# A seven-product MLP: the first batch's tokens one step earlier, and another order of the products in a unit

## The reference

```python
# attention, 8 heads of 64: local window |i-j| < 16, plus 24 block summaries (max of k, mean of v)
a = softmax([mask(q k^T / 8), q k_sum^T / 8 + log 32]);  x = a @ [v, v_sum]
# gated convolution ("MoE" in the names): w_in 512 x 1024, 3 taps, w_out 1024 x 512
h = relu(x @ w_in);  c = conv3(h, conv_w) over tokens;  x = (h * sigmoid(c)) @ w_out
# layer norm and MLP: w_ch1 512 x 2048, w_ch2 2048 x 512
xn = (x - mean) / sqrt(var + 1e-6) * g_ln;  out = x + relu(xn @ w_ch1) @ w_ch2
```

## Time and profile before

| | |
|---|---|
| median of three runs | 494.68 us |
| profiled execution | 494.09 us |
| its span, first to last instruction | 492.4 us |
| TensorE busy | 472.2 us (96%), 2807 matmuls |
| VectorE busy | 288.1 us (59%) |
| ScalarE busy | 213.8 us (43%) |
| GpSimd busy | 275.3 us (56%) |
| chain that ended last | TensorE 80%, VectorE 10% |

### The profile page before, as it was taken

How to read it: one execution, slowest core, us unless ns; L and a number is a source line. 1 busy time by engine, 2 the same in 40 slices (tenths; PEclk the granted TensorE clock), 3 DMA queues, 4 the chain that set the end, 5 groups by cost and what they waited for, 6 DMA issues and landing times.

```text
span 492.4 us, 7970 instructions
## 1 busy us (share of the span) xinstructions
PE 472.2 (96%) x2807; PEld 416.4 (85%) x2807; DVE 288.1 (59%) x616; ACT 213.8 (43%) x516; POOL 275.3 (56%) x413
## 2 busy tenths in 40 slices
PE   7978899999999999997999999999999999999996
PEld 7866777898989898876889898888998988888985
DVE  6498987488756785898655334165573334243324
ACT  3878988834334545634434234333410313231310
POOL 3447788999801300577786787784005187787300
PEclk9999999999999999999999999999999999999999
DMA  9999981121100200000120222022020022102003
GB/s 221 222 236 209 225 204 57 47 85 47 40 0 1 86 1 0 1 0 28 60 87 4 82 86 86 2 86 85 2 107 23 0 87 85 62 25 88 0 1 128
DMA packets 62115, 35.63 MB, mean 72 GB/s; under 512 B 48064, under 2 KB 55004, under 8 KB 61788
## 3 DMA queue, kind: packets, MB, share of 16 engines
q1 hardware_dynamic: 60508, 34.72, 25.6%
q10 hardware_dynamic: 1568, 0.39, 0.4%
HBM read 31.08 MB, written 3.15 MB: 70 GB/s over the span
## 4 chain that ended last, share of the span: by engine, by line
PE 80%; DVE 10%; SPq 3%; issue 2%; POOL 2%; DMA 1%; ACT 1%; DVEq 0%; POOLq 0%
PE two L1375 10%; PE two L1377 9%; PE two L1376 9%; PE two L1352 7%; PE two L1355 7%; PE two L1354 7%; PE two L1215 4%; PE two L1217 4%; PE two L1216 4%; PE two L1281 4%; PE two L1282 4%; PE two L1283 4%; PE two L1167 2%; PE two L1156 2%; DVE h L778 2%
## 5 line engine op out<-in xcount | busy, mean ns | idle before, releaser
L1375 PE MATMUL two<-wv,h 128*128 128x512 f32 x192 | 77.0, 401 | 2.9 <-DVE h L778 2.7
L1355 PE MATMUL two<-combo,wa 128*128 128x384 f32 x224 | 75.6, 337 | 0.0
L1352 PE MATMUL two<-combo,wa 128*128 128x384 f32 x224 | 75.5, 337 | 0.0
L1354 PE MATMUL two<-combo,wa 128*128 128x384 f32 x224 | 75.3, 336 | 0.0
L1377 PE MATMUL two<-wv,h 128*128 128x512 f32 x192 | 75.2, 392 | 0.0
L1376 PE MATMUL two<-wv,h 128*128 128x512 f32 x192 | 75.2, 392 | 0.0
L582 POOL TENSOR_TENSOR wa<-wst,wa 128x256 fp32r<-128x256 f32 x39 | 31.4, 835 | 54.4 <-ACT wa L1006 54.4
L540 POOL TENSOR_TENSOR wa<-asum,wa 128x256 fp32r<-128x256 f32 x52 | 44.6, 859 | 4.3
L1375 PEld LDWEIGHTS two<-wv,h 128*128 128x128 f32 x192 | 36.0, 188 | 13.0 <-DVE h L778 6.6
L546 POOL TENSOR_TENSOR asum<-wst 128x256 f32<-128x256 f32 x26 | 22.9, 881 | 43.0 <-PE two L1355 32.0
L851 DVE TENSOR_TENSOR u<-two,u 128x384 f32<-128x384 f32 x16 | 8.9, 558 | 64.9 <-PE two L1355 64.9
(11 more groups left out here) (120 smaller groups left out, 1041.8 us busy)
## 6 DMA issues: line engine op xcount, KB each, us to landing
wst<-in_moe_w_ch SPq DMA_DIRECT2D x26, 512.0 KB, 3.4
vW<-in_v SPq DMA_DIRECT2D x16, 240.0 KB
kn<-in_k SPq DMA_DIRECT2D x15, 192.0 KB, 4.0
qn<-in_q SPq DMA_DIRECT2D x15, 192.0 KB, 3.7
out<-y SPq DMA_DIRECT2D x11, 256.0 KB, 2.0
vblk<-in_v SPq DMA_DIRECT2D x3, 768.0 KB, 6.4
wst<-in_moe_w_in SPq DMA_DIRECT2D x8, 256.0 KB, 3.5
wst<-in_moe_w_out SPq DMA_DIRECT2D x8, 256.0 KB, 2.9
```

Source lines behind the costliest of these rows:

```text
L1352: nc.tensor.matmul(o, wk[:, 0, kk], ck[:, 0, kk], start=(first and kk == 0), stop=False, skip_group_check=True)
L1354: nc.tensor.matmul(o, wk[:, 0, kk], ck[:, 1, kk], start=False, stop=False, skip_group_check=True)
L1355: ins = nc.tensor.matmul(o, wk[:, 1, kk], ck[:, 0, kk], start=False, stop=(kk == 1), skip_group_check=True)
L1375: nc.tensor.matmul(o, hi, vh, start=(f == 0 and c == 0), stop=False, skip_group_check=True)
```

## The change

The first batch's tokens are transposed in steps 11 and 12, not 12 and 13; centring stands in front of gate(10). The first batch's token sums are VectorE's, in step 12, and its `combo` tiles are spread over steps 12 to 14, with a wait of its own for `combo3`. In a unit TensorE's order becomes products 0 to 2, tiles 0 to 2, products 3 and 4, tiles 3 to 5, products 5 and 6; in the last unit tiles 3 to 5 stand behind product 6. `h2_low(g, 1)` stands in front of the sum of `p1`; tokens of the second batch are behind tiles 1 and 2; `stats`, `copy_y`, the second batch's `combo` tiles and `add_out` move to fit.

```diff
--- before.py
+++ after.py
@@ -65,12 +65,12 @@
         COLS_STEP = GPP * (NPAIR - 2)
 
 
-        TOK_TILE = {12: {0: 0, 1: 1, 3: 2, 4: 3}, 13: {0: 4, 1: 5, 3: 6, 4: 7}}
-        TOK_UNIT = {2: {3: 0, 4: 1}, 3: {3: 2, 4: 3}, 4: {3: 4, 4: 5}, 5: {3: 6, 4: 7}}
+        TOK_TILE = {11: {0: 0, 1: 1, 3: 2, 4: 3}, 12: {0: 4, 1: 5, 3: 6, 4: 7}}
+        TOK_UNIT = {2: {1: 0, 2: 1}, 3: {1: 2, 2: 3}, 4: {1: 4, 2: 5}, 5: {1: 6, 2: 7}}
         NSLOT = 2 * KD
 
 
-        COMBO_ORDER = [(0, 2, 6, 3, 1, 4, 5), (0, 1, 2, 3, 4, 5, 6)]
+        COMBO_ORDER = [(0, 2, 6, 1, 3, 4, 5), (0, 1, 2, 3, 4, 5, 6)]
         SUMS = {3: ((1, 0),), 4: ((1, 1),), 6: ((2, 0),), 9: ((2, 1),), 12: ((3, 0),), 15: ((3, 1),)}
         place = [0]
 
@@ -551,13 +551,6 @@
 
                     pool.wait_ge(x_done, NG)
                 elif l == 1:
-                    for i in range(4):
-                        out, in0, in1, op = token_sum(i)
-                        if i == 0:
-                            pool.wait_ge(xr_done, NSLOT)
-                        else:
-                            pool.wait_ge(tsum_done, i)
-                        nc.gpsimd.tensor_tensor(out, in0, in1, op).then_inc(tsum_done, 1)
 
                     pool.wait_ge(h_ready, 4 * KF)
                 elif l == 2:
@@ -787,23 +780,24 @@
             for s in range(2 * KF):
                 if s >= 1:
                     taps(s)
+                    if s == KF + 2:
+                        inverse_std(0)
+                        dve.wait_ge(rstd_done, 1)
+                        for i in range(T):
+                            centre(0, i)
                     gate(s)
                 if s == KF + 1:
                     for i in range(T):
                         stats(i)
-                if s == KF + 2:
-                    inverse_std(0)
-                    dve.wait_ge(rstd_done, 1)
-                    for i in range(T):
-                        centre(0, i)
-                if s == 2 * KF - 3:
+                elif s == KF + 4:
+                    token_sums(0, range(4))
+                elif s == KF + 5:
                     for k in COMBO_ORDER[0][0:3]:
                         combo_low(0, k)
-                if s == 2 * KF - 2:
-                    for k in COMBO_ORDER[0][3:5]:
+                elif s == KF + 6:
+                    for k in COMBO_ORDER[0][3:6]:
                         combo_low(0, k)
-            for k in COMBO_ORDER[0][5:7]:
-                combo_low(0, k)
+            combo_low(0, COMBO_ORDER[0][6])
 
             dve.wait_ge(hg_done, 2 * KF)
             for g in range(NU):
@@ -811,27 +805,33 @@
                 dve.wait_ge(p1_done, g + 1)
                 dve.wait_ge(prod_done, NPROD * g + 2)
                 nc.vector.tensor_tensor(u2[:], b, p1[:], ALU.add).then_inc(u2_done, 1)
-                if g == 1:
-                    for i in range(4):
-                        stats(T + i)
-                elif g == 2:
+                if g == 2:
                     inverse_std(1)
                     dve.wait_ge(rstd_done, 2)
                     for i in range(3):
                         centre(1, i)
+                elif g == NFP + 1:
+                    add_out(5)
+                h2_low(g, 0)
+                if g == 1:
+                    for i in range(4):
+                        stats(T + i)
                 elif g == 6:
                     token_sums(1, (0, 1))
                 elif g == NFP - 1:
-                    combo_low(1, 0)
-                    combo_low(1, 1)
+                    for k in range(3):
+                        combo_low(1, k)
                 elif g == NFP:
-                    for k in (4, 5, 6):
-                        combo_low(1, k)
-                elif g == NFP + 1:
-                    add_out(5)
-                h2_low(g, 0)
+                    combo_low(1, 5)
+                    combo_low(1, 6)
+                    add_out(0)
+                    add_out(1)
                 dve.wait_ge(prod_done, NPROD * g + 4)
                 nc.vector.tensor_tensor(u3[:], b, p1[:], ALU.add).then_inc(u3_done, 1)
+                dve.wait_ge(prod_done, NPROD * g + 5)
+                dve.wait_ge(u3_done, g + 1)
+                nc.vector.tensor_tensor(u3[:], a, u3[:], ALU.add).then_inc(c22_done, 1)
+                h2_low(g, 1)
                 if g == 1:
                     for i in range(4, T):
                         stats(T + i)
@@ -841,21 +841,18 @@
                 elif g == 6:
                     token_sums(1, (2, 3))
                 elif g == NFP - 1:
-                    combo_low(1, 2)
                     combo_low(1, 3)
+                    combo_low(1, 4)
                 elif g == NFP:
-                    for n in range(5):
+                    for n in range(2, 5):
                         add_out(n)
-                dve.wait_ge(prod_done, NPROD * g + 5)
-                dve.wait_ge(u3_done, g + 1)
-                nc.vector.tensor_tensor(u3[:], a, u3[:], ALU.add).then_inc(c22_done, 1)
                 dve.wait_ge(prod_done, NPROD * g + 6)
                 nc.vector.tensor_tensor(p1[:], b, p1[:], ALU.add).then_inc(c21_done, 1)
                 dve.wait_ge(prod_done, NPROD * g + 7)
                 dve.wait_ge(u2_done, g + 1)
                 nc.vector.tensor_tensor(u2[:], a, u2[:], ALU.add).then_inc(c12_done, 1)
-                for k in (1, 2, 3):
-                    h2_low(g, k)
+                h2_low(g, 2)
+                h2_low(g, 3)
             for n in range(T, NTT):
                 add_out(n)
 
@@ -986,6 +983,8 @@
                     act.wait_ge(prod_done, NPROD * (NFP * b - 1) + k + 1)
                 elif k == 5:
                     act.wait_ge(h_ready, 4 * KF)
+                elif k == 3:
+                    act.wait_ge(h_ready, 2 * (KF + 6))
                 else:
                     act.wait_ge(tile_proj, T * (KF + 3))
                 nc.scalar.copy(combo[k][:, 0], combo_src(k)).then_inc(ch_done, 1)
@@ -1040,6 +1039,8 @@
                 at_tile = TOK_TILE.get(s, {})
                 if s >= 1:
                     tap0(s)
+                    if s == KF + 2:
+                        root(0)
                     for i in (0, 1, 3):
                         if i in at_tile:
                             tokens(0, at_tile[i], ps_h[at_tile[i] % 2])
@@ -1052,16 +1053,13 @@
                 if s == KF + 1:
                     for n in range(T):
                         copy_y(n)
-                if s == KF + 2:
-                    root(0)
-                if s == 2 * KF - 3:
+                if s == KF + 4:
                     for i in COMBO_ORDER[0][0:3]:
                         combo_high(0, i)
-                if s == 2 * KF - 2:
-                    for i in COMBO_ORDER[0][3:5]:
+                elif s == KF + 5:
+                    for i in COMBO_ORDER[0][3:6]:
                         combo_high(0, i)
-            for i in COMBO_ORDER[0][5:7]:
-                combo_high(0, i)
+            combo_high(0, COMBO_ORDER[0][6])
             raw_high(1)
 
             act.wait_ge(hg_done, 2 * KF)
@@ -1074,20 +1072,16 @@
                     act.wait_ge(h2_done, 4 * g)
                 nc.scalar.copy(p1[:], a[:, 0:HALF]).then_inc(p1_done, 1)
                 if g == 0:
-                    for n in range(T, T + 3):
-                        copy_y(n)
+                    copy_y(T)
                 elif g == 2:
                     root(1)
-                elif g == NFP - 1:
-                    combo_high(1, 0)
-                    combo_high(1, 1)
                 h2_high(g, 0)
                 if g == 0:
-                    for n in range(T + 3, NTT):
+                    for n in range(T + 1, T + 4):
                         copy_y(n)
                 elif g == NFP - 1:
-                    combo_high(1, 2)
-                    combo_high(1, 3)
+                    for i in range(3):
+                        combo_high(1, i)
                 for i in sorted(slots):
                     tokens(1, slots[i], a)
                 for l in range(1, NLOAD):
@@ -1096,11 +1090,17 @@
                             raw_high(l)
                         v2_high(l)
                 h2_high(g, 1)
+                if g == 0:
+                    for n in range(T + 4, NTT):
+                        copy_y(n)
+                elif g == NFP - 1:
+                    combo_high(1, 3)
+                    combo_high(1, 4)
                 h2_high(g, 2)
                 h2_high(g, 3)
                 if g == NFP - 1:
-                    for i in (4, 5, 6):
-                        combo_high(1, i)
+                    combo_high(1, 5)
+                    combo_high(1, 6)
 
 
         @block.tensor
@@ -1390,19 +1390,21 @@
                     tokens_t(1, TOK_UNIT[g][i], ps_h[g % 2])
 
             for g in range(NU):
-                product(g, 0)
-                product(g, 1)
+                for k in range(3):
+                    product(g, k)
                 for i in range(3):
```

(10 more changed lines are left out.)

## The result

The changed kernel is slower: 498.23 us against 495.67, medians of eleven runs each, ratio 1.0056 with a 95% interval of 1.0036 to 1.0075, so 2.8 us (1.8 to 3.7). The forecast was 4.0 more, 498.7, counted from a median of 494.68; eleven runs of the kernel before put that median at 495.67. The profiled execution took 497.33 us, 3.24 more than the one of before, and its span is 495.6. Both parts of the forecast are in the trace: all the old waits have gone, and 15 new ones have come.

What follows compares the result with a forecast made beforehand. TensorE was taken to bound the kernel, the span being its matmuls plus pauses. Savings -10.5, added wait +14.0 and tokens +0.5 gave +4.0 us, so a median of 498.7 us; range 493.3 to 502.

Steps and rivals of the forecast that it cites:

- Savings, 10.5: TensorE's old pauses at the MLP's start, its end and the unit boundaries go: 10.5 us saved in all.
- Start of the MLP: Waits for hg in project(14) and before project(15), and product 3's 0.25 in unit 0, go: -4.5 us.
- End: Wait of 1.58 us before the last unit's tiles goes, covered by three held tiles: -1.8 us.
- Boundaries: Late first tiles of units, beside GpSimd, become ready long before, with three products in front: -4.2 us.
- The added wait, 14.0: Product 2 waits at each unit boundary for the copy to p1, behind VectorE's h2 lows: 14.0 us added (8.2 to 18).
- The quiet pause: Product 2's pause at boundaries with GpSimd idle (6-7, 9-10, 14-15): 0.41 us, 0.5 with the slower first matmul.
- Unit 8: Boundary 7-8: two combo copies stand before the p1 copy in ScalarE's queue; product 2 pauses 1.1 us.
- Small edits: Moved tokens, centring, combo, add_out, copy_y and stats: nothing, except the second batch's tokens in unit 2, 0.5 us late.
- the lock in full: Rival: boundary lows take 1.1 us or more each beside GpSimd, 18 us added, 502 to 504; chance 0.10 with the late hg case.
- The covered case: Rival: p1 is there in time at boundaries, only the savings remain: -10.5 us, 484 to 486; chance 0.08.
- the late front: Rival: hg 15 late again at the MLP's start, beside load 1's raw sums, 0 to 2 us more; chance 0.10, shared.
- The quiet case: Rival: GpSimd misses the boundary lows or slows few: 8.2 us added instead of 14.0, 492.9 to 495.7; chance 0.24.

Runs made afterwards that it cites:

- e3: Kernel before with only the first batch's part: tokens in steps 11 and 12, sums on VectorE, combo tiles over steps 12 to 14; 490.65 us, ratio 0.9876.
- e4: Kernel before with only tiles 3 to 5 of the last unit held until behind product 6; 494.86 us, ratio 0.9968 to the kernel before.
- e2: Changed kernel with product 2 behind tile 0 (products 0, 1, tile 0, product 2, tiles 1, 2); 486.78 us, ratio 0.9808 to the kernel before.
- e1: Changed kernel with ScalarE's copy to p1 waiting for three lows, not four, and VectorE waiting before writing u2; 489.06 us, ratio 0.9847 to the kernel before.
- e6: Changed kernel with h2_low(g, 1) moved back behind product 6, in front of lows 2 and 3; 513.94 us, ratio 1.0350 to the kernel before.
- e7: Changed kernel with product 2 behind tile 0 and the second batch's square root moved from unit 2 to unit 1; 485.46 us, ratio 0.9793 to the kernel before.

## Why the prediction was right

**Savings, 10.5.** About right in each term. Start of the MLP: 1.09 + 0.10 + 2.95 + 0.11, and 0.26 behind `u2`, gone (e3 alone: 4.6 us of pauses less). End: 1.86 gone (e4 alone: 1.4 there, as its own order put 0.39 and 0.08 in the place, and 0.2 at the boundaries; the changed order, with three tiles between product 2 and product 4, has no such pause). Boundaries: 4.2, gone (e2, too).

**The added wait, 14.0.** Right in place, chain and releaser (e1 removes it by one count, e6 lengthens it by one low), and 1.1 too high in size. The terms: 11 boundaries at 0.95 became nine at 0.87; 4-5 at 0.54, where GpSimd was at work too but both lows took 0.55; and 0-1 at 0.55, where another 0.3 stands in front of product 0 (below). That is 1.6 less. I had taken both lows as slowed at each boundary; in the second batch (10-11 to 13-14) it was the second alone, 0.55 and 0.89 each time, as at 419.05 above, and at 8-9 both were slowed but took only 0.73 and 0.72 (pause 0.70). The quiet pause was sized at 0.41 and measured 0.51 to 0.54: I took 0.05 from the end of the copy to TensorE's start. That is what the trace of before shows behind an instruction of VectorE. This low ends at 480.79, and the tile of the earlier trace rows, which waits for it, starts at 480.84:

```profile
480.24 0.55 DVE L778 SCALAR_TENSOR_TENSOR h<-p,h 128x384 fp32r<-128x384 f32 x1
```

Behind ScalarE it is 0.15 (470.48 to 470.63), and the same at each of the 15 pauses. Unit 8: 1.1 forecast, 1.19 measured.

**Small edits.** Tokens of unit 2: 0.5 forecast, 0.83 measured. With product 2 behind tile 0 the same wait is 1.42, and moving the square root takes 0.92 of that (e7), so its place is most of it there. Missed: product 0 of unit 1 starts 0.21 late (0.3 with refill), at 233.56. It waits for the sum of `p1`, which VectorE starts at 232.87, directly behind low 1 (232.14); and low 1 waited for its high part, which ScalarE made at 231.58, behind `copy_y` and `v2_high`. I had put what is late in unit 0 inside the boundary's 0.95.

The sum with measured terms is -10.5 + 12.9 + 0.8 + 0.3 = +3.5, less 0.2 by which the attention ended earlier in this execution: 3.3, where the profiled times differ by 3.24. That the median of 498.23 lies within 0.5 of the forecast's 498.7 is partly luck: the forecast was counted from 494.68, and the kernel before came out 1.0 above that. The added time was 2.8 (1.8 to 3.7) where 4.0 was forecast, and the wait's size and the two small terms are off in opposite directions. Two of the prediction's sums also mix their starting points: an added 12 to 17 gives 496.7 to 501.7 from the median, and the lock in full 502.7 to 504.7.

**The rivals.** The covered case fell with the 15 waits, the late front with the missing waits for `hg`. The quiet case, at 8.2 added, lies further from the measured 12.9 than the forecast's 14.0; it was nearer than I made it by one boundary, 4-5; 0-1 is at the quiet level too, but only because its product 0 was late. What I gave as a reason for it was misread for unit 6: the last two lows ran at 0.55 in units 2 to 5 of before, but in unit 6 the first of them took 1.64.

The lock in full fell as I had priced it: of the 30 lows at the boundaries none took more than 1.10 us, and their mean is 0.70. But its mechanism is in the trace. In the changed kernel 26 of the lows that read `p1`, `u2` or `u3` began with more than 0.15 us of a GpSimd operation still to run, and each ended 0.40 to 0.42 behind the end of that operation, 25 such lows of the kernel before likewise. The Trainium skill's rule (SBUF — State Buffer, "Who interferes with whom": exclusive, the later one waits) agrees with this, and with the way round seen at 419.05, where VectorE kept 0.55 and GpSimd took the 0.40. So the low waits for what is left of GpSimd's operation, not for a whole one, and a low that comes first doesn't wait; a partly used lock was the wrong reading of 0.75 to 1.10, and so was that both lows wait at each boundary. The longest lows, 1.49 to 1.60 in units 2 to 6, are those of block 1 beside GpSimd's operations of 1.3 us (263.14 is the first); they stand in front of product 5, where TensorE didn't wait for them.

## What to carry to other kernels

When an operation moves forward in its queue, work out the release of every semaphore that it waits for, not only of those that the move was about: what stood in front of it was a cover. If the chain behind one of them is too long, first look whether the wait counts more than the data needs; here one count was worth 10.8 us. Moving two parts together hid that one of them, alone, was worth 1% (e3) and the rest cost more than that.

## What the runs showed of the hardware

- From the end of ScalarE's instruction to the start of the matmul that it releases are 0.15 us (15 pauses of the changed kernel), from VectorE's 0.05 (six waits of the kernel before).
- VectorE's low with two SBUF inputs takes 0.55 us when GpSimd is idle. When a GpSimd operation is already running, the low ends 0.40 to 0.42 us behind the end of that operation: it took 0.60 to 1.10 at the boundaries, up to 1.60 beside operations of 1.3 us. When VectorE's began first, as at 419.05, it took 0.55 and GpSimd's operation 1.14 instead of 0.74.
- The low of block 0, which reads one of TensorE's banks and only one SBUF tile, took 0.54 to 0.56 us in all 16 units of the changed kernel, also where it ran beside GpSimd (238.14, 273.01).
- With pauses up to 1.2 us in each unit of 17 us the granted clock stayed at the 2.4 GHz level throughout the MLP. In e6, with nine pauses of 1.8 to 2.1 us, it fell behind two of them, of 2.05 and 2.04, to the 1.2 GHz level (0.57 on average over 3.5 to 4 us, matmuls on 384 columns 0.32 apart instead of 0.17), and not behind the longest, 2.08. Each fall cost 1.6 us, so the cost of a pause isn't only its length.
